# Gated product on groups of 128 tokens behind a top-k attention: x stationary, weights moving 384 columns at a time

## The chip, the core and the metric

The kernel runs on one NeuronCore of a Trainium2 chip. The metric is the device time of one execution in microseconds (us), as a median of several runs. The engines are TensorE (PE; its weight loads are listed as PEld), VectorE (DVE), ScalarE (ACT), GpSimd (POOL) and SyncE (SP, which here only starts DMAs).

## What is computed

```
q, k, v: (4, 8, 576, 64) f32      w_a, w_b: (512, 1536)      w_out: (1536, 512)

scores = q @ k.T / 8                                  # per batch and head, 576 x 576
kth = the 32nd largest score of each row
attn = softmax(scores where scores >= kth, else -1e9)
o = attn @ v                                          # (4, 8, 576, 64)
x = o with heads side by side                         # (2304 tokens, 512)
out = ((x @ w_a) * (x @ w_b)) @ w_out                 # (2304, 512)
```

All matrix products but those with the probabilities use operands split in a high and a low part of type fp32r, and three products (high x high, high x low, low x high) are added in PSUM.

## The kernel before, in words

**Attention.** The work comes in 72 units. A unit is one tile of 128 queries for one pair of heads (`p`, 4 pairs in each of 4 batches), or, for the last 64 queries of a batch, the tail tile of two pairs at once; there are 8 such tail units. `ORDER` gives the order of the tiles in each batch. For each unit, TensorE transposes q (L434), makes the scores in two halves (`qk`, L462), VectorE finds the 32 largest values of each row by four rounds of MAX8 and three of MATCH_REPLACE8 (L887, L904) and writes the mask `keep` (L919). GpSimd adds the mask (L810), ScalarE takes exponentials (L655) and normalises (L670), TensorE transposes the row of both heads in a part of 4 and a part of 5 blocks (`transposes`, L484), multiplies with v (`probs_v`, L501), and subtracts the high part of x to get the low one (L512). Keys of a pair are split and transposed in two parts, `preps` (L420), in the slots that `PREP_SLOT` names.

**Slots.** Each engine runs one loop over slots `s`, in an order of work written out by hand: in slot s, TensorE does `probs_v` of unit s-2, queries of unit s+2, scores of unit s+1, and the transposes of unit s-1, while VectorE searches unit s. The steps of the gated product stand between these.

**The product.** Tokens are taken in 9 groups of G = 256. A group is ready when its 8 units are done, so the product begins in slot `MOE0` = 9. For each of 12 blocks F of 128 hidden columns there are three steps: "a" and "b" (L536: the weight block of 128 x 128 is stationary, x of 256 tokens moves, 4 blocks of the model dimension x 3 = 12 matmuls of 256 columns each) give a and b with the hidden dimension on the partitions; "o" (L551: two halves of the tokens x 3 = 6 matmuls of 512 columns) adds h @ w_out into two PSUM banks. Between them ScalarE copies a and b out of PSUM (L694), GpSimd multiplies (L816), ScalarE rounds to `h_hi` (L699), GpSimd subtracts to `h_lo` (L820). The slots hold 4 and 5 steps by turns (`steps_of`); what is left of the 330 steps after the last slot runs in a loop of its own behind it, and there the engines have nothing else.

```
n = 4 * (s - MOE0) + (s - MOE0) // 2
todo = [[n + part - HALF_SLOT] for part in range(4)] + [[n + 4 - HALF_SLOT] if (s - MOE0) % 2 == 1 else []]
```

**Weights.** There are 36 parts of 128 x 512 (`WCH`): 12 of w_a, 12 of w_b, 12 of w_out. In slots 0 to 9, four per slot, SP loads each to `stage`, ScalarE rounds it to `w_hi` (L604), GpSimd subtracts to the low part (L789). The first 18 low parts stay in SBUF (`w_lo`); the low parts of the last two row blocks of w_b and of all of w_out go to a scratch in memory (`store_low`, L336) and come back for every use: `wb_lo` (128 KB per block F, L351) and `wo_lo` (256 KB per F, L343), in rings of two buffers. The same ring `wo_lo` serves the low parts on their way out.

Of the kernel before, what the change touches and what calls it, by code (L numbers as in the profile page):

```python
# [6 lines left out]
def topk_attention_gated_product(nc, q, k, v, w_parts, xs, out):  # L7
# [3 lines left out]
    P = 128  # L11
# [22 lines left out]
    G = 256  # L34
    GT = G // P
    GROUPS = TOKENS // G
    WC = 512
    WCH = w_parts.shape[0]
    WB0 = KB * DFF // WC
    WO0 = 2 * WB0  # L40

# [4 lines left out]
    RING = 2  # L46
    RING_B = 2
# [6 lines left out]
    ORDER = [[0, 1, 2, 3, 4], [0, 4, 1, 2, 3], [0, 1, 2, 4, 3], [4, 0, 1, 2, 3]]  # L54
# [22 lines left out]
    FIRST, LAST = 0, NU + 2  # L77
    NPREPS = 2 * KB * BATCHES
    PREP_SLOT = [-1] * 4 + [p - 2 for p in range(2, KB) for part in range(2)]
    for b in range(1, BATCHES):  # L80
        late = NU
        slots = []
        for p in range(KB - 1, -1, -1):
            n = b * KB + p - KPAIRS
            free = last_unit(n // KB, n % KB) - 1 if n >= 0 else 0
            for part in range(2):
                at = min(first_unit(b, p) - 2, late - 1)
                if at < free:
                    at = late
                slots.append(at)  # L90
                late = at
        PREP_SLOT += slots[::-1]

# [13 lines left out]
    for b in range(1, BATCHES):  # L107
        for p in range(KB):
            V_AT.setdefault(last_unit(b - 1, p) + 3, []).append((b, p))


    NFS = NF * GROUPS
    STEPS = []
    for F in range(NFS + 2):
        STEPS += [("a", F), ("b", F), ("o", F - 2)]
    MOE0 = PER + 1
    MOE_END = LAST
    PARTS = 5
    HALF_SLOT = 2

    def steps_of(s):

        n = 4 * (s - MOE0) + (s - MOE0) // 2
        todo = [[n + part - HALF_SLOT] for part in range(4)] + [[n + 4 - HALF_SLOT] if (s - MOE0) % 2 == 1 else []]
        return [[m for m in part if m >= 0] for part in todo] if s >= MOE0 else [[]] * PARTS

    SLOT_OF = {n: s for s in range(FIRST, MOE_END) for part in steps_of(s) for n in part}
    N_SLOTTED = len(SLOT_OF)

    def o_step(F):  # L130
        return 3 * (F + 2) + 2


    STAGES = 3
    W_AT = [(0, 1), (0, 3)] + [(s, part) for s in range(1, MOE0 + 1) for part in range(4)]
    W_AT = W_AT[:WCH]
    W_SLOTS = W_AT[-1][0] + 1

    def w_of(s, part):
        return [W_AT.index((s, part))] if (s, part) in W_AT else []  # L140

# [4 lines left out]
    with ExitStack() as ctx:  # L146
# [8 lines left out]
        wo_lo = sb("wo_lo", [P, RING, WC], fp32r)  # L155
        wb_lo = sb("wb_lo", [P, RING_B, KB - LKB, P], fp32r)
        stage = sb("stage", [P, STAGES, WC])
        y = stage
# [18 lines left out]
        ab = sb("ab", [P, 2, 2, G])  # L177
        h_hi = sb("h_hi", [P, 2, G], fp32r)
        h_lo = sb("h_lo", [P, 2, G], fp32r)
# [4 lines left out]
        BY = 4  # L184
        ps_ab = ps[:, 6, :].rearrange("p (w t) -> p w t", w=2)
        ps_x = ps[:, 7, :]
# [6 lines left out]
        def keys_in_psum(n):  # L193
            return [ps_45, ps_67, ps_67, ps_t][n] if n < 4 else ps_t
# [23 lines left out]
        ld_wb = [sem(f"ld_wb{n}") for n in range(RING_B)]  # L218
        ld_wo = [sem(f"ld_wo{n}") for n in range(RING)]
        st_wo = [sem(f"st_wo{n}") for n in range(RING)]  # L220
# [29 lines left out]
        ab_done = sem("ab_done")  # L250
        ab_copied = sem("ab_copied")
        h_ready = sem("h_ready")
        h_hi_ready = sem("h_hi_ready")
        h_lo_ready = sem("h_lo_ready")
# [18 lines left out]
        for g in range(GROUPS):  # L273
            pieces = []
            for t in range(GT):
                tokens = TOKEN_OF[g * G + t * P:g * G + (t + 1) * P]
                at = 0
                while at < P:
                    n = 1
                    while at + n < P and tokens[at + n] == tokens[at] + n:  # L280
                        n += 1
                    pieces.append((t, at, n, tokens[at]))
                    at += n
            PIECES.append(pieces)
# [5 lines left out]
        def _(sp):  # L290
# [37 lines left out]
            def load_w(c):  # L328
                if c < WCH:
                    wait(sp, w_lo_done, c - STAGES + 1)  # L330
                    sp.dma_start(stage[:, c % STAGES, :], w_parts[c]).then_inc(ld_w[c % STAGES], 16)

            def store_low(c):
                n = c - LOW
                sp.wait_ge(w_lo_done, c + 1)
                sp.dma_start(xs[n * P:(n + 1) * P, :], wo_lo[:, n % RING, :].bitcast(fp32)  # L336
                             ).then_inc(st_wo[n % RING], 16)

            def load_wo(F):
                wait(sp, o_done, F - RING + 1)  # L340
                f = F % NF
                row = (WO0 - LOW + f) * P
                sp.dma_start(wo_lo[:, F % RING, :].bitcast(fp32), xs[row:row + P, :]  # L343
                             ).then_inc(ld_wo[F % RING], 16)

            def load_wb(F):
                wait(sp, ab_done, F - RING_B + 1)
                f = F % NF
                at = f % (WC // P) * P
                parts = xs[0:(WO0 - LOW) * P, :].rearrange("(k b p) c -> b p k c", k=KB - LKB, p=P)  # L350
                sp.dma_start(wb_lo[:, F % RING_B, :, :].bitcast(fp32), parts[f // (WC // P), :, :, at:at + P]  # L351
                             ).then_inc(ld_wb[F % RING_B], 16)

            def store_y(g):
                wait(sp, y_ready, GT * (g + 1))
                for t, at, n, row in PIECES[g]:
                    sp.dma_start(out[row:row + n, :], y[at:at + n, t, :]).then_inc(st_y, 16)

            def after_step(n):
                F = n // 3  # L360
                if n % 3 == 1 and F + RING_B < NFS:
                    load_wb(F + RING_B)
                F = n // 3 - 2
                if n % 3 == 2 and F >= 0:
                    if F + RING < NFS:
                        load_wo(F + RING)
                    if F % NF == NF - 1:
                        store_y(F // NF)
# [7 lines left out]
            for c in range(STAGES):  # L376
                load_w(c)
# [3 lines left out]
            for s in range(FIRST, LAST):  # L381
                for b, p in V_AT.get(s, []):
                    load_v(b, p)
                load_q(s + 4)
                mine = preps_at(s)
                for part in range(PARTS):
                    for n in steps_of(s)[part]:
                        after_step(n)
                    if part in (2, 3) and len(mine) > part - 2:
                        load_k(mine[part - 2] + 2)  # L390
                    for c in w_of(s, part):
                        if c >= LOW:
                            store_low(c)
                        load_w(c + STAGES)
                if s == MOE0 - 1:
                    for n in range(RING):
                        sp.wait_ge(st_wo[n], 16 * ((WO0 - LOW) // RING))
                    for F in range(RING_B):
                        load_wb(F)
# [569 lines left out]
```

## Time and profile before

| | us |
|---|---|
| median of 3 runs | 875.44 (873.91 to 876.31) |
| time of the profiled execution | 875.8 |
| its span, first to last instruction | 874.0 |
| TensorE busy | 814.9 (93%) |
| VectorE busy | 780.9 (89%) |
| ScalarE busy | 623.4 (71%) |
| GpSimd busy | 455.5 (52%) |
| mean granted clock of TensorE | 0.969 of full speed |

Busy time of TensorE overstates its load, since matmuls overlap in the pipeline: the distance from one start to the next is what a matmul costs in a row of them. The chain that ended last is followed back from the last instruction to what released each step.

### The profile page before, as it was taken

How to read it: one execution, taken by the hardware profiler on the slowest of the kernel's cores; microseconds unless marked ns; L12 is line 12 of the kernel's file. 1: busy time of each engine (PE TensorE's matmuls, PEld its weight loads, DVE VectorE, ACT ScalarE, POOL GpSimd, SP SyncE). 2: the span in 40 equal slices, each digit the busy share in tenths (PEclk: the TensorE clock that was granted, in tenths of full speed). 3: DMA queues.
4: the chain of work that ended last, by engine and by line, in shares of the span. 5: the costliest groups of instructions: out<-in, count | busy, mean ns of one | idle time of the engine just before them, and what ended most of it. 6: DMA issues, size and time to landing. Idle time of an engine off the chain costs nothing.

```text
span 874.0 us, 19133 instructions
## 1 busy us (share of the span) xinstructions
PE 814.9 (93%) x6576; PEld 734.0 (84%) x6576; DVE 780.9 (89%) x1663; ACT 623.4 (71%) x1416; POOL 455.5 (52%) x504
## 2 busy tenths in 40 slices
PE   6666679999999999999999999999999999999997
PEld 4455568889899998898899999898999998898996
DVE  7899999998999999999999999999999999995000
ACT  5787777777877777778777777787777777775222
POOL 2677754555544455555554455655445445544332
PEclk9966689999999999999999999999999999999999
DMA  4635552222522232224422322233323222311332
GB/s 124 152 110 164 194 164 56 75 75 75 147 80 68 73 97 74 73 80 128 107 77 73 91 68 74 73 106 89 95 74 103 68 68 68 91 55 56 109 91 85
DMA packets 133520, 81.48 MB, mean 93 GB/s; under 512 B 82736, under 2 KB 110384, under 8 KB 133424
## 3 DMA queue, kind: packets, MB, share of 16 engines
q1 hardware_dynamic: 132880, 80.12, 33.0%
q8 instruction: 54, 0.88, 0.4%
q14 instruction: 42, 0.34, 0.1%
q10 hardware_dynamic: 544, 0.13, 0.1%
HBM read 70.78 MB, written 9.44 MB: 92 GB/s over the span
## 4 chain that ended last, share of the span: by engine, by line
DVE 51%; PE 31%; issue 10%; ACT 4%; POOL 2%; DMA 1%; SPq 0%; ACTq 0%
DVE work L904 25%; DVE best L887 20%; PE ps L536 12%; PE ps L551 6%; DVE keep L919 6%; PE ps L462 3%; PE ps L501 3%; PE ps L484 2%; PE ps L420 2%; POOL scores L810 2%; PE ps L434 1%; ACT scores L670 1%; ACT q_t L635 1%; DMA k_rows_b<-in_k 1%; PE ps L442 0%
## 5 line engine op out<-in xcount | busy, mean ns | idle before, releaser
L887 DVE MAX8 best<-work 128x8 f32<-128x576 f32 x432 | 304.7, 747 | 0.0
L536 PE MATMUL ps<-x_hi,w_hi 128*128 128x256 f32 x864 | 251.4, 291 | 0.9 <-ACT x_lo L688 0.9
L810 POOL TENSOR_TENSOR scores<-scores,keep 128x576 f32<-128x576 f32 x144 | 214.7, 1510 | 58.5 <-DVE keep L919 58.5
L536 PE MATMUL ps<-x_lo,w_hi 128*128 128x256 f32 x864 | 243.2, 281 | 0.0
L904 DVE MATCH_REPLACE8 work<-best,work 128x576 f32<-128x576 f32 x288 | 212.8, 743 | 0.0
L536 PE MATMUL ps<-x_hi,w_lo 128*128 128x256 f32 x648 | 182.4, 281 | 0.0
L536 PEld LDWEIGHTS ps<-x_hi,w_hi 128*128 128x128 f32 x864 | 163.0, 189 | 2.2 <-ACT x_lo L688 1.4
L820 POOL TENSOR_TENSOR h_lo<-ab,h_hi 128x256 fp32r<-128x256 f32 x108 | 81.0, 750 | 158.5 <-ACT h_hi L699 158.5
L536 PEld LDWEIGHTS ps<-x_lo,w_hi 128*128 128x128 f32 x864 | 163.2, 189 | 0.5
L655 ACT ACTIVATE scores<-scores,neg_max 128x576 f32<-128x576 f32 x144 | 111.9, 778 | 68.0 <-POOL scores L810 67.2
L462 PE MATMUL ps<-k_t,q_t 128*128 128x288 f32 x632 | 121.2, 320 | 4.9 <-ACT scores L643 4.9
L678 ACT COPY probs_t<-ps 128x512 f32<-128x512 f32 (+1 forms) x144 | 93.4, 649 | 42.2 <-PE ps L484 42.1
L536 PEld LDWEIGHTS ps<-x_hi,w_lo 128*128 128x128 f32 x648 | 122.0, 188 | 0.0
L816 POOL TENSOR_TENSOR ab<-ab 128x256 f32<-128x256 f32 x108 | 80.2, 743 | 75.7 <-ACT ab L694 75.6
L484 PE MATMUL ps<-ident,scores 128*128 128x128 f32 x648 | 100.3, 284 | 20.2 <-ACT probs_t L678 12.8
L670 ACT ACTIVATE scores<-scores,inverse 128x576 f32<-128x576 f32 x144 | 113.5, 788 | 3.1 <-DVE inverse L914 2.1
L694 ACT COPY ab<-ps 128x512 f32<-128x512 f32 x108 | 63.4, 587 | 68.6 <-PE ps L536 67.9
L501 PE MATMUL ps<-probs_t,v_rows 128*64 128x128 f32 (+1 forms) x1600 | 103.7, 282 | 9.1 <-ACT probs_t L678 9.1
L501 PEld LDWEIGHTS ps<-probs_t,v_rows 128*64 128x64 f32 x1600 | 85.8, 145 | 28.1 <-ACT probs_t L678 12.4
L643 ACT COPY scores<-ps 128x576 f32<-128x576 f32 x142 | 92.4, 651 | 18.9 <-PE ps L462 16.6
L904 DVE MATCH_REPLACE8 work<-best,scores 128x576 f32<-128x576 f32 x144 | 105.8, 742 | 0.0
L887 DVE MAX8 best<-scores 128x8 f32<-128x576 f32 x144 | 101.8, 747 | 3.3 <-ACT scores L647 3.3
(56 smaller groups left out, 1294.4 us busy)
## 6 DMA issues: line engine op xcount, KB each, us to landing
wo_lo<-x_scratch SPq DMA_DIRECT2D x108, 256.0 KB, 2.7
wb_lo<-x_scratch SPq DMA_DIRECT2D x108, 128.0 KB, 2.2
stage<-in_w SPq DMA_DIRECT2D x36, 256.0 KB, 3.0
q_rows<-in_q SPq DMA_DIRECT2D x142, 64.0 KB, 2.3
x_scratch<-wo_lo SPq DMA_DIRECT2D x18, 256.0 KB, 2.8
v_rows<-in_v SPq DMA_DIRECT2D x32, 128.0 KB, 2.4
out<-stage SPq DMA_DIRECT2D x15, 256.0 KB, 2.7
k_rows_a<-in_k SPq DMA_DIRECT2D x16, 128.0 KB, 2.3
```

The source lines that it names most:

```text
L462: last = mm(ps_s[:, j, :], weights, k_t[:, (b * KB + p) % KPAIRS, at:at + HALF], start=(i == 0), stop=(i == len(terms) - 1))
L484: last = tr(ps_t[:, at - a:at - a + P], row_of(u)[:, at:at + P], ident[:])
L501: last = mm(ps_x[h * D:(h + 1) * D, i * w:(i + 1) * w], v_rows[:, p, block, h * D:(h + 1) * D], probs_t[:, at:at + w], start=(i == 0 and c ...
L536: last = mm(ps_ab[:, which, :], w, x[:, g % 2, kb, :], start=(kb == 0 and i == 0), stop=(kb == KB - 1 and i == 2))
L643: A.copy(scores[:, u % ROWS, :, half * HALF:(half + 1) * HALF], ps_s[:]).then_inc(s_ready, 1)
L655: A.activation(row, row, ACT.Exp, bias=neg_max[:, u % 2, j:j + 1], scale=SCALE, accum_out=sums[:, u % 2, j:j + 1]).then_inc(e_ready, 1)
L670: A.mul(row, row, inverse[:, u % 2, j:j + 1]).then_inc(p_ready, 1)
L678: A.copy(probs_t[:, a:z], ps_t[:, 0:z - a]).then_inc(pt_ready, 1)
L810: V.tensor_tensor(row, row, keep[:, j, :], ALU.add).then_inc(mask_done, 1)
L820: V.tensor_tensor(h_lo[:, (F - 1) % 2, :], ab[:, (F - 1) % 2, 0, :], h_hi[:, (F - 1) % 2, :], ALU.subtract).then_inc(h_lo_ready, 1)
L887: ins = V.max(best[:, u % 2, j, 8 * r:8 * r + 8], src)
L904: V.match_replace(out=work[:, j, :], in_to_replace=best[:, u % 2, j, 8 * r:8 * r + 8], in_values=src, imm_value=NEG).then_inc(chain, 1)
```

## The change

The product works on 18 groups of 128 tokens. The hidden columns are taken in 4 chunks of HC = 384 per group, 72 chunks in all (`NCH`), and exactly one chunk belongs to a slot, beginning with slot `MOE0` = 5 and ending in slot 78. x (128 tokens) is stationary, 384 columns of the weights move, and so a and b come out with tokens on the partitions. Their product must therefore be turned for the last product: three transposes of 128 x 128 on TensorE (`turn_hidden`), from SBUF to PSUM; ScalarE copies the result twice, once rounded to `h_hi`, once as it is to `h`, and GpSimd subtracts. The output of a chunk (`output`) is 9 matmuls of 512 columns into one PSUM bank, two slots after its columns.

In slot s, with n = s - MOE0, TensorE does the output of chunk n-2 at the head of the slot, half of the a columns of chunk n between the two halves of the scores, the other half after the keys, turns chunk n-1, transposes the first part of the probabilities, does the b columns of chunk n, and transposes the second part. All keys of a slot are transposed together, before the second half of the a columns. GpSimd multiplies chunk n-1 right after the masks, then does up to five weight splits, and the remainder `h_lo` of chunk n-1 last.

`wo_lo` and `wb_lo` become one buffer each, of 768 KB and 384 KB per chunk; low parts on their way to memory have two buffers of their own (`leaving`). `stage` has four buffers in place of three. The weights are split in the order in which chunks need them (`W_ORDER`), five per slot in slots 2 to 4 and four in slots 5 to 8. `ORDER` and `PREP_SLOT` are changed: tail units are units 16 to 19 and 52 to 55 (before: 16, 17, 22, 23, 48, 49, 54, 55), and two slots more than before prepare two key parts each.

```diff
-    G = 256
+    G = P
+    HC = 384
+    HB = HC // P
+    NH = DFF // HC
+    NCH = GROUPS * NH
...
-    RING = 2
-    RING_B = 2
-    ORDER = [[0, 1, 2, 3, 4], [0, 4, 1, 2, 3], [0, 1, 2, 4, 3], [4, 0, 1, 2, 3]]
+    ORDER = [[0, 1, 2, 3, 4], [4, 0, 1, 2, 3], [0, 1, 2, 3, 4], [4, 0, 1, 2, 3]]
...
+        PREP_SLOT += [at + n for n in ((-5, -4, -3, -3, -2, -2, -1, -1) if b % 2 else (-6, -5, -4, -3, -2, -1, 0, 1))]
...
+    MOE_END = MOE0 + NCH + 2
+    for cb in range(NCB):
+        W_BASE.append(len(W_ORDER))
+        W_ORDER += [WB0 + kb * NCB + cb for kb in range(LKB, KB)] + [kb * NCB + cb for kb in range(KB)]
+        W_ORDER += [WB0 + kb * NCB + cb for kb in range(LKB)]
+        last = NF if cb == NCB - 1 else (cb + 1) * HB
+        W_ORDER += [WO0 + f for f in range(cb * HB, last)]
+    STAGES = 4
+    W_AT = [(0, 2), (0, 4)] + [(1, m) for m in (0, 1, 2, 4)] + [(s, m) for s in range(2, 5) for m in range(5)]
+    W_AT += [(s, m) for s in range(5, 9) for m in (0, 1, 2, 4)]
...
+            def load_wo(n):
+                wait(sp, o_done, n)
+                if n < NH:
+                    stored_until(W_ORDER.index(WO0 + f + HB - 1))
...
+            def load_wb(n):
+                wait(sp, ab_done[1], n)
...
+            def columns_of(n, which, blocks):
+                if blocks[0] == 0:
+                    wait(pe, ab_copied[which], n)
+                    if n < NH:
+                        pe.wait_ge(w_lo_done, W_BASE[columns_need(n) - 1] + [KB - LKB + KB, 2 * KB][which])
+                if which == 0:
+                    wait(pe, xlo_done, PER * g + (3 if blocks[0] == 0 else PER))
+                for kb in blocks:
...
+                    for m, (x, w) in enumerate(((x_hi, high), (x_hi, low), (x_lo, high))):
+                        last = mm(ps_ab[which], x[:, g % 2, kb, :], w,
+                                  start=(kb == 0 and m == 0), stop=(kb == KB - 1 and m == 2))
...
+            def turn_hidden(n):
+                pe.wait_ge(h_ready, n + 1)
+                wait(pe, ht_copied, n)
+                for b in range(HB):
+                    last = tr(ps_h[:, b * P:(b + 1) * P], ab[:, 0, b * P:(b + 1) * P], ident[:])
...
+            def output(n):
+                pe.wait_ge(h_lo_ready, n + 1)
+                pe.wait_ge(ld_wo, 16 * (n + 1))
+                for b in range(HB):
+                    for m, (x, w) in enumerate(((h_hi, high), (h_hi, wo_lo[:, b, :]), (h_lo, high))):
+                        last = mm(ps_y, x[:, cols], w, start=(f + b == 0 and m == 0), stop=(f + b == NF - 1 and m == 2))
...
+                output(n - 2)
                 probs_v(s - 2)
                 q_transposes(s + 2)
                 qk(s + 1, 0)
-                steps(todo[1])
+                columns_of(n, 0, (0, 1))
                 x_subtract(s - 2)
                 q_subtract(s + 2)
                 qk(s + 1, 1)
...
+                for m in mine:
+                    k_transposes(m)
+                columns_of(n, 0, (2, 3))
+                turn_hidden(n - 1)
                 transposes(s - 1, 0)
+                columns_of(n, 1, (0, 1, 2, 3))
                 transposes(s - 1, 1)
...
+            def copy_hidden(n):
+                A.copy(h_hi[:], ps_h).then_inc(h_hi_ready, 1)
+                wait(act, h_lo_ready, n)
+                A.copy(h[:], ps_h).then_inc(ht_copied, 1)
...
                 masked(s - 1, 0)
                 masked(s - 1, 1)
                 shifts(s)
+                hidden(n - 1)
+                for m in range(2, 5):
+                    weights(s - 1, m)
+                weights(s, 0)
...
+                weights(s, 1)
+                hidden_lo(n - 1)
```

## Rows read from the trace of the kernel before

**Rows 1.** The page: busy time, bytes moved in 40 slices, the chain.

```profile
PE 814.9 (93%) x6576; PEld 734.0 (84%) x6576; DVE 780.9 (89%) x1663; ACT 623.4 (71%) x1416; POOL 455.5 (52%) x504
...
GB/s 124 152 110 164 194 164 56 75 75 75 147 80 68 73 97 74 73 80 128 107 77 73 91 68 74 73 106 89 95 74 103 68 68 68 91 55 56 109 91 85
...
DVE 51%; PE 31%; issue 10%; ACT 4%; POOL 2%; DMA 1%; SPq 0%; ACTq 0%
```

**Rows 2.** Windows: stretch, its length, busy us per engine (instructions), granted clock, DMA.

```profile
66.00:113.00 47.00, 30.27 (x169) 23.75 (x169) 47.00 (x96) 36.09 (x80) 34.09 (x29) 0.64 0.58 186
...
636.00:798.00 162.00, 160.87 (x1344) 146.38 (x1345) 162.00 (x354) 118.93 (x274) 81.29 (x92) 1.00 0.26 74
798.00:874.00 76.00, 68.20 (x477) 62.28 (x473) 0.27 (x2) 21.44 (x46) 24.74 (x32) 0.98 0.30 87
```

**Rows 3.** Groups of instructions: busy us, mean ns of one, idle before.

```profile
L810 POOL TENSOR_TENSOR scores<-scores,keep 128x576 f32<-128x576 f32 x144 | 214.7, 1510 | 58.5 <-DVE keep L919 58.5
...
L820 POOL TENSOR_TENSOR h_lo<-ab,h_hi 128x256 fp32r<-128x256 f32 x108 | 81.0, 750 | 158.5 <-ACT h_hi L699 158.5
...
L694 ACT COPY ab<-ps 128x512 f32<-128x512 f32 x108 | 63.4, 587 | 68.6 <-PE ps L536 67.9
...
L789 POOL TENSOR_TENSOR wo_lo<-stage,w_hi 128x512 fp32r<-128x512 f32 x18 | 22.8, 1277 | 11.9 <-DMA x_scratch<-wo_lo 8.9 <-ACT w_hi L604 2.9
```

**Rows 4.** Timeline of VectorE, the masks of units 8, 29, 33, 37, 63, 71: start, length.

```profile
111.61 1.94 DVE L919 TENSOR_SCALAR keep<-scores,best 128x576 f32<-128x576 f32 x2
...
342.07 0.93 DVE L919 TENSOR_SCALAR keep<-scores,best 128x576 f32<-128x576 f32 x2
...
385.98 1.76 DVE L919 TENSOR_SCALAR keep<-scores,best 128x576 f32<-128x576 f32 x2
...
430.71 1.08 DVE L919 TENSOR_SCALAR keep<-scores,best 128x576 f32<-128x576 f32 x2
...
712.66 0.94 DVE L919 TENSOR_SCALAR keep<-scores,best 128x576 f32<-128x576 f32 x2
...
797.16 0.95 DVE L919 TENSOR_SCALAR keep<-scores,best 128x576 f32<-128x576 f32 x2
```

**Rows 5.** Timeline of TensorE through two plain units.

```profile
704.69 1.31 PE L501 MATMUL ps<-probs_t,v_rows 128*64 128x128 f32 x20
...
708.13 0.22 PE L512 MATMUL ps<-x_hi,neg_ident 128*128 128x128 f32 x1
...
708.36 0.69 PE L462 MATMUL ps<-k_t,q_t 128*128 128x288 f32 x4
...
710.31 0.60 PE L484 MATMUL ps<-ident,scores 128*128 128x128 f32 x4
710.66 0.36 PE L536 MATMUL ps<-x_hi,w_hi 128*128 128x256 f32 x1
...
717.67 0.28 PE L512 MATMUL ps<-x_hi,neg_ident 128*128 128x128 f32 x1
...
718.43 0.80 PE L462 MATMUL ps<-k_t,q_t 128*128 128x288 f32 x4 [0.15 <-ACT scores L643]
...
725.81 0.33 PE L501 MATMUL ps<-probs_t,v_rows 128*64 128x128 f32 x2
```

**Rows 6.** Timeline of TensorE, key transposes in a slot that prepares keys.

```profile
416.34 0.77 PE L420 MATMUL ps<-ident,k_rows_a 128*128 128x128 f32 x5 [0.51 <-ACT q_t L635]
```

**Rows 7.** Timeline of TensorE in the tail.

```profile
831.04 0.28 PE L536 MATMUL ps<-x_hi,w_hi 128*128 128x256 f32 x1
...
833.91 0.40 PE L551 MATMUL ps<-w_hi,h_hi 128*128 128x512 f32 x1
...
835.31 0.28 PE L536 MATMUL ps<-x_hi,w_hi 128*128 128x256 f32 x1
...
868.11 0.47 PE L551 MATMUL ps<-w_hi,h_hi 128*128 128x512 f32 x1 [1.44 <-DMA wo_lo<-x_scratch]
```

**Rows 8.** DMA issues: transfer, count, size, us to landing.

```profile
wo_lo<-x_scratch SPq DMA_DIRECT2D x108, 256.0 KB, 2.7
```

More of the change, by code:

```diff
@@ L73, in last_unit @@
         return max(u for u in range(NU) if UNITS[u][0] == b and p in UNITS[u][2])
-    FIRST, LAST = 0, NU + 2
+    FIRST = 0
     NPREPS = 2 * KB * BATCHES
-    PREP_SLOT = [-1] * 4 + [p - 2 for p in range(2, KB) for part in range(2)]
+    PREP_SLOT = [-1] * 4 + [0, 0, 1, 1]
     for b in range(1, BATCHES):
[L81 to L92, printed above, removed]
+        at = first_unit(b, 0)
+        PREP_SLOT += [at + n for n in ((-5, -4, -3, -3, -2, -2, -1, -1) if b % 2 else (-6, -5, -4, -3, -2, -1, 0, 1))]
+    for n in range(2 * KB, NPREPS):
+        b, p, before = n // 2 // KB, n // 2 % KB, n // 2 - KPAIRS
+        assert PREP_SLOT[n] <= first_unit(b, p) - 2
+        assert before < 0 or PREP_SLOT[n] >= last_unit(before // KB, before % KB) - 1
     def preps_at(s):
@@ L274, in topk_attention_gated_product @@
             pieces = []
[L275 to L283, printed above, removed]
+            tokens = TOKEN_OF[g * G:(g + 1) * G]
+            at = 0
+            while at < G:
+                n = 1
+                while at + n < G and tokens[at + n] == tokens[at] + n:
+                    n += 1
+                pieces.append((at, n, tokens[at]))
+                at += n
             PIECES.append(pieces)
@@ L339, in load_wo @@
[L339 to L352, printed above, removed]
@@ L354, in store_y, with load_w @@
-            def store_y(g):
[L355 to L368, printed above, removed]
+            def load_w(i):
+                if i < WCH:
+                    wait(sp, w_lo_done, i - STAGES + 1)
+                    sp.dma_start(stage[:, i % STAGES, :], w_parts[W_ORDER[i]]).then_inc(ld_w[i % STAGES], 16)
@@ new lines, in stored_until @@
+            def stored_until(last):
+                for n in range(LOWS):
+                    wait(sp, st_w[n], 16 * sum(LEAVING[m] <= last for m in range(n, len(LEAVING), LOWS)))
+            def load_wo(n):
+                if not 0 <= n < NCH:
+                    return
+                wait(sp, o_done, n)
+                f = n % NH * HB
+                if n < NH:
+                    stored_until(W_ORDER.index(WO0 + f + HB - 1))
+                sp.dma_start(wo_lo[:].bitcast(fp32), xs_o[f * P:(f + HB) * P, :].rearrange("(b p) c -> p b c", p=P)
+                             ).then_inc(ld_wo, 16)
@@ L370, in _, with weights @@
+            def weights(s, m):
+                for i in w_of(s, m):
+                    if W_ORDER[i] >= LOW:
+                        store_low(i)
+                    load_w(i + STAGES)
             load_k(0)
@@ L375, in _ @@
             load_q(2)
-            for c in range(STAGES):
-                load_w(c)
+            load_w(0)
+            load_w(1)
             load_k(4)
@@ L417, in k_transposes @@
                 if n >= 2:
-                    wait(pe, kt_ready, n)
+                    wait(pe, kt_ready, n if to is ps_t else n - 1)
+                if n >= 4 and to is not ps_t:
+                    wait(pe, ab_copied[1], PREP_SLOT[n] - MOE0)
                 for b in range(NB - part):
@@ L755, in _ @@
                 copy_scores(s + 1, 0)
-                between(s, 1)
+                weights(s, 1)
                 normalise(s - 1, 0)
@@ L836, in _ @@
                 split_k(n)
-            for s in range(FIRST, LAST):
+            for s in range(FIRST, MOE_END):
                 masked(s - 1, 0)
```

382 lines of the change are left out of this document (169 added, 213 removed).

## The prediction

> **What bounds the kernel now.** I read the page first, then busy time by stretch, then the timelines of VectorE and TensorE, then the tail. The page [rows 1] shows two engines that are nearly full, TensorE at 93% of the span and VectorE at 89%, and the chain gives 51% of the span to VectorE and 31% to TensorE. So neither is the limit throughout. The windows [rows 2] split the span in three parts with different limits.
>
> The first part ends at about 113 us. From 66 to 113 us TensorE is only 30 of 47 us busy and its granted clock averages 0.64 of full, so between its levels of 1.2 and 2.4 GHz, since there is no product work yet. VectorE is full. GpSimd splits the weights.
>
> The second part ends with the last comparison, `keep` of unit 71, at 797.16 + 0.95 = 798.1 us [rows 4]. From 712.66 to 797.16 eight units take 84.50 us, 10.56 us each, and no gap stands between VectorE's instructions: this is its floor per unit. Over the eight units from 342.07 to 430.71, in which keys are prepared, a unit takes 11.08 us. Over the whole 63 units from 111.61 it is 10.88, some 20 us above the floor, and all of these 20 us lie in the stretches that prepare keys or hold tail units.
>
> Is TensorE far from being the limit in a plain unit? Two units go from 704.69 to 725.81, 21.12 us [rows 5]. Its starts there follow each other without a hole but for one place: from the subtraction of x (L512) to the second half of the scores (L462) it takes 0.76 us from 717.67, and 0.23 from 708.13, where nothing is late, and the scores after it lose another 0.12. That is 0.65 us of waiting for ScalarE. So a plain unit holds (21.12 - 0.65) / 2 = 10.24 us of TensorE work, 0.3 us under VectorE's floor. That small margin is what the change spends.
>
> The third part is the tail: 874.0 - 798.1 = 75.9 us, with VectorE idle and TensorE 68.2 of 76 us busy [rows 2]. The product is late there: 4.5 of its steps fit in a unit from unit slot 9 on, so some 40 of 330 steps are left over after the last slot, nine slots' worth.
>
> **The change part by part.** *The width.* Per slot the product does today 1.5 blocks of 128 hidden columns on 256 tokens: 36 matmuls of 256 columns and 9 of 512. After, it is 24 of 384, the same 9 of 512, and 3 transposes. In the tail, starts go from 831.04 to 833.91 for 24 matmuls of 256, 119.6 ns each, and to 835.31 for six of 512, 233 ns each [rows 7]. A matmul of 384 I put midway, 176.5 ns; in proportion to either neighbour it would be 175 to 179. So 36 x 0.1196 = 4.31 us becomes 24 x 0.1765 = 4.24, within -0.11 and 0. Each matmul has a weight load of its own before (6576 of each [rows 1]), and still has. A transpose of 128 by 128 in fp32 takes 0.35 / 4 = 0.088 us (four from 710.31 to 710.66 [rows 5]), three 0.26. The sum is +0.19 us: 10.43 us per plain unit against VectorE's 10.56. The margin of 0.3 becomes 0.1.
>
> The Trainium skill ("TensorE: Matmul & The Clock Gate", Back-to-back issue gap) gives N/2.4 + 2.5 ns for a warm matmul, 162.5 ns at 384 columns. By it the slot would be 0.3 us lighter than I reckon. At 256 it gives 109 where the tail shows 119.6, so I keep the rows.
>
> *The tail.* A group of 128 tokens is ready after 4 units, so the product starts in slot 5, not 9, and goes one chunk per slot: 72 chunks end their columns in slot 76 and their output in slot 78. From the last `keep` at D: slot 72 waits for masks, exponentials and normalising of unit 71 as now (its transposes start about D+6), and ends about D+9.1; slot 73 has output 2.1, probabilities times v 1.24, columns 4.24, turning 0.26 and about 0.7 of waits and switches, to D+17.7. Slots 74 to 76 hold 4.24 + 2.1 + 0.26 plus 0.4 of waits, 7.0 each, to D+38.8. Then output of chunk 70 (2.1), the load of `wo_lo` for chunk 71, its output (2.1), the copy (0.6) and the store (2.7), with 0.5 of hand-overs. `wo_lo` now has one buffer, and a load brings 768 KB only after the output before it. One of 256 KB lands in 2.7 us [rows 8], and already keeps TensorE waiting 1.44 us at the end [rows 7]; 768 KB lies between that and three times it, 8.1. I take 4.9: the bytes at the page's best slice, 194 GB/s, need 4.0, and something is fixed. That gives D+51, against D+75.9 now: -25 us. With 2.7 us it is -27, with 8.1, four times 3.2 more, -12.
>
> *The start.* All slots from 5 to 8 now carry product work and weight splits together. GpSimd per slot: two masks of 1.51, four splits of about 1.28, and product and remainder of 384 columns, each 1.5 x 0.75 = 1.1 [rows 3], with 0.2 for the shift: 10.5 us, before any wait. Lows that leave for memory go through two buffers, and each must be stored before it is reused. I take 12.1 us per slot in place of some 11.2: +3.6. Slots 2 to 4 hold five splits in place of four, 9.6 us of GpSimd: +1. Chunk 2 needs 28 weight parts at a time when GpSimd is just doing the 28th, and `wo_lo` for chunks 2 and 3 can load only when splits 33 and 36 have been stored, one slot before it is used: +3. Part of chunk 0 runs at the low clock, with 3.6 us of matmuls more to pay twice at worst: +1.5. Sum +9, bounds 0 (all of it under VectorE) and +20.
>
> *The slots with keys or tail units*, about 24 after slot 12. TensorE bounds them, so +0.19 is paid in full. The cover between the two halves of the scores falls from a step of 1.4 us to half a column job of 1.06, and key transposes already waited 0.51 us for ScalarE's copy of q [rows 6]; I add 0.1. 24 x 0.3 = +7, bounds -2 and +12.
>
> *The other 39 slots* fit under VectorE by 0.1 us. I charge 0.1 each for what does not fit, +4, bounds 0 and +16.
>
> *Hidden at nothing:* ScalarE copies 384 columns four times per slot where it copied 1.5 x 512 and 1.5 x 256, about +0.4 us, on an engine 71% busy. If it came on the chain, it would be in the 39 slots' upper bound. DMA traffic for lows doubles (384 to 768 KB of `wo_lo` and 192 to 384 KB of `wb_lo` per slot), at a DMA share of 0.26 [rows 2]. q, k and v queue behind it on SP, and are asked for two slots or more ahead.
>
> Sum: 874.0 - 25 + 9 + 7 + 4 = 869.0 us of span. The profiled execution took 875.8, 1.8 more than its span and 0.4 above the median of the runs; so 870.4, rounded to 870.
>
> **The rivals.** *A. TensorE bounds every slot.* The margin of 0.1 us is smaller than one handover, and outputs now wait within the same slot for turning, two copies and a remainder. If a plain slot costs 0.35 us over my sum, 39 of them cost 14 us: 884. For it: TensorE is 160.9 of 162 us busy from 636 to 798 [rows 2]. Against: the output's chain (copies 0.8, remainder 1.1) has 3 us of other work over it. It decides from 0.2 us per slot on; it is the case on the other side.
>
> *B. GpSimd and VectorE collide.* A pair of `keep` takes 0.93 to 0.95 us alone and 1.76 at 385.98 us [rows 4], in a stretch where GpSimd works at that time. The remainder of a chunk now comes last before the masks, just when VectorE compares. If it lands on `keep` in each plain slot, half of that, 0.4 x 39 = 16 us: 886. Against: the second half of the scores can start 4.8 us after a `keep` ends (718.43 against 712.66 + 0.94); then 0.52, half a column job 1.06 and turning 0.5 bring 6.9, ScalarE is free for the two copies about 7.4 and done at 8.2, the remainder ends at 9.3, and the next `keep` begins at 9.6. So it fits by 0.3 us if TensorE isn't late, and B mostly follows A. The Trainium skill ("SBUF — State Buffer", Who interferes with whom) says that a tensor_scalar in a two-port mode and a GpSimd instruction exclude each other for the whole instruction; the trace agrees with its 1.76, and by that rule one collision could cost up to 1.1 us.
>
> *C. Everything hides.* The start costs 3, the key slots 0, the rest 0: 874.0 - 25 + 3 + 1.4 = 853. For it: VectorE has been full in the first part and GpSimd has gaps there.
>
> *D. The gain and the costs cancel:* a start at +14, or loads of 768 KB near 8 us: 875.
>
> **How the numbers follow.** My forecast (863 to 872.8) 0.42, C and what lies between 0.12, D (872.8 to 878) 0.15, A and B 0.31. A measurement of this kernel tells 0.3%, 2.6 us, from no change. Faster 0.54, the same 0.15, slower 0.31. The range runs from 856, near C, to 887, which takes in A and B.
>
> **What would show it.** Right: the last `keep` 15 to 25 us later than 798 and the span's end about 51 us behind it; matmuls of 384 columns 175 to 179 ns apart; slots 5 to 9 over 12 us; plain slots of 10.6 to 10.7. Wrong: plain slots of 11 us with `keep` pairs of 1.3 us and more (A, B), outputs in the tail waiting over 5 us for `wo_lo`, or `keep` 8 at no more than 115 us (C).

## The result and the profile after

The changed kernel takes 865.22 us (864.08 to 867.99, 4 runs) against 875.38 for the kernel before, a ratio of 0.989 with a 95% interval of 0.9862 to 0.9918. The forecast was 870, faster, with a range of 856 to 887. So the change gains 1.1%, clear of the noise and inside the range. The profiled execution has a span of 862.2 us against 874.0, so 11.8 us less.

The page after: busy time per engine and the chain. They answer to [rows 1].

```profile
PE 814.6 (94%) x5928; PEld 734.1 (85%) x5928; DVE 781.6 (91%) x1663; ACT 660.3 (77%) x1488; POOL 442.9 (51%) x432
...
DVE 51%; PE 25%; issue 11%; DMA 4%; ACT 3%; POOL 3%; SPq 1%; ACTq 0%; POOLq 0%
```

Windows after, to hold against [rows 2]: length, busy us of PE, PEld, DVE, ACT, POOL, granted clock, DMA.

```profile
66.00:111.00 45.00, 38.25 (x269) 34.05 (x270) 43.62 (x93) 38.08 (x88) 36.43 (x33) 0.92 0.69 216
118.00:121.00 3.00, 3.00 (x8) 2.32 (x8) 2.59 (x7) 0.34 (x3) 1.62 (x2) 0.50 0.42 158
650.00:810.00 160.00, 159.63 (x1179) 145.30 (x1178) 159.41 (x345) 126.27 (x286) 79.24 (x77) 1.00 0.43 129
810.00:862.20 52.20, 43.34 (x246) 37.08 (x244) 0.17 (x1) 16.08 (x37) 14.23 (x14) 0.96 0.43 136
```

VectorE's masks after, units 8, 9, 10, 23, 24, 29, 33, 34, 70 and 71: start, length. They answer to [rows 4].

```profile
110.42 1.96 DVE L923 TENSOR_SCALAR keep<-scores,best 128x576 f32<-128x576 f32 x2
123.31 0.94 DVE L923 TENSOR_SCALAR keep<-scores,best 128x576 f32<-128x576 f32 x2
137.84 0.93 DVE L923 TENSOR_SCALAR keep<-scores,best 128x576 f32<-128x576 f32 x2
...
284.80 1.70 DVE L923 TENSOR_SCALAR keep<-scores,best 128x576 f32<-128x576 f32 x2
296.14 1.20 DVE L923 TENSOR_SCALAR keep<-scores,best 128x576 f32<-128x576 f32 x2
...
349.24 0.92 DVE L923 TENSOR_SCALAR keep<-scores,best 128x576 f32<-128x576 f32 x2
...
393.80 1.69 DVE L923 TENSOR_SCALAR keep<-scores,best 128x576 f32<-128x576 f32 x2
405.12 1.69 DVE L923 TENSOR_SCALAR keep<-scores,best 128x576 f32<-128x576 f32 x2
...
797.92 0.93 DVE L923 TENSOR_SCALAR keep<-scores,best 128x576 f32<-128x576 f32 x2
808.48 0.93 DVE L923 TENSOR_SCALAR keep<-scores,best 128x576 f32<-128x576 f32 x2
```

And GpSimd's remainder `h_lo` (L842) beside the masks of units 34 and 70:

```profile
405.42 1.07 POOL L842 TENSOR_TENSOR h_lo<-h,h_hi 128x384 fp32r<-128x384 f32 x1 [4.51 <-ACT h L728]
...
796.58 1.02 POOL L842 TENSOR_TENSOR h_lo<-h,h_hi 128x384 fp32r<-128x384 f32 x1 [4.45 <-ACT h L728]
```

These rows give the sum. The last mask ends at 809.4 us, 11.3 later than before (798.1). Behind it stand 862.2 - 809.4 = 52.8 us, where 75.9 stood: 23.1 less. And 11.3 - 23.1 is the -11.8. Of the 11.3 us, 4.1 are lost by the mask of unit 10 (137.84 against 133.75 before), and 7.2 in all the units after it. Most plain units still take 10.56 us (808.48 - 797.92): VectorE's floor has not moved. There the remainder is done before the masks begin (796.58 + 1.02 against 797.92). A unit in the stretch with keys takes 11.32 (405.12 - 393.80); the remainder runs inside its mask pair, which takes 1.69 us. Some plain units are long too: 11.34 us from unit 23, with a pair of 1.70, to unit 24.

TensorE in a plain slot after: two runs of a columns, the second half of the scores, the turning (L557), transposes, b columns. It answers to [rows 5] and [rows 7].

```profile
729.15 0.34 PE L546 MATMUL ps<-w_hi,x_hi 128*128 128x384 f32 x1
...
730.26 0.33 PE L451 MATMUL ps<-q_t,neg_ident 128*128 128x256 f32 x1
...
730.95 0.34 PE L546 MATMUL ps<-w_hi,x_hi 128*128 128x384 f32 x1
...
732.00 0.49 PE L557 MATMUL ps<-ident,ab 128*128 128x128 f32 x3
732.33 0.60 PE L493 MATMUL ps<-ident,scores 128*128 128x128 f32 x4
732.69 0.42 PE L546 MATMUL ps<-w_hi,x_hi 128*128 128x384 f32 x1
...
740.77 0.33 PE L451 MATMUL ps<-q_t,neg_ident 128*128 128x256 f32 x1
```

Six matmuls of 384 columns start at 730.95 and the next work at 732.00: 175 ns each, near the 176.5 put in the sum. The same instruction comes back 10.51 us later (730.26, 740.77), and no start in between waits. TensorE's work in a plain slot is thus 10.5 us, 0.05 under VectorE's floor, where I had reckoned 10.43.

TensorE's waits for `wo_lo`, in slot 9 and for the last output, and the transfer itself (size, median us to landing; compare [rows 8]).

```profile
114.04 0.74 PE L493 MATMUL ps<-ident,scores 128*128 128x128 f32 x5
117.70 0.66 PE L574 MATMUL ps<-w_hi,h_hi 128*128 128x512 f32 x1 [2.92 <-DMA wo_lo<-x_scratch]
118.16 0.63 PE L574 MATMUL ps<-wo_lo,h_hi 128*128 128x512 f32 x1
118.58 0.63 PE L574 MATMUL ps<-w_hi,h_lo 128*128 128x512 f32 x1
...
855.42 0.76 PE L574 MATMUL ps<-w_hi,h_hi 128*128 128x512 f32 x1 [4.45 <-DMA wo_lo<-x_scratch]
```

```profile
wo_lo<-x_scratch SPq DMA_DIRECT2D x72, 768.0 KB, 4.7
```

The wait of 2.9 us costs twice: after it the matmuls of the output start 0.43 us apart (118.16, 118.58) where they are 0.23 apart at full clock. TensorE was at its lower level, 1.2 GHz, until about 121 us: the granted clock over 118 to 121 us is 0.50, and over 111 to 125 us it averages 0.88.

### The profile page after: what moved, and what is told of

Read it like the earlier page. It is cut to its first block, busy times and chain, and to the rows that moved or that the text cites. A ratio compares the mean times of both kernels' runs of the same rounds, so it can differ in the third digit from the quotient of the medians.

```text
span 862.2 us, 18109 instructions
## 1 busy us (share of the span) xinstructions
PE 814.6 (94%) x5928; PEld 734.1 (85%) x5928; DVE 781.6 (91%) x1663; ACT 660.3 (77%) x1488; POOL 442.9 (51%) x432
## 4 chain that ended last, share of the span: by engine, by line
DVE 51%; PE 25%; issue 11%; DMA 4%; ACT 3%; POOL 3%; SPq 1%; ACTq 0%; POOLq 0%
DVE work L908 25%; DVE best L891 20%; PE ps L546 9%; DVE keep L923 6%; PE ps L574 6%; PE ps L471 3%; PE ps L511 3%; DMA wo_lo<-x_scratch 2%; PE ps L493 2%; POOL scores L828 2%; PE ps L429 2%; POOL leaving L803 1%; PE ps L443 1%; DMA x_scratch<-leaving 1%; PE ps L557 1%
## 5 line engine op out<-in xcount | busy, mean ns | idle before, releaser
L842 POOL TENSOR_TENSOR h_lo<-h,h_hi 128x384 fp32r<-128x384 f32 x72 | 77.5, 1077 | 348.0 <-ACT h L728 348.0
L546 PE MATMUL ps<-w_hi,x_hi 128*128 128x384 f32 x576 | 203.2, 353 | 0.6 <-ACT x_lo L708 0.6
L546 PE MATMUL ps<-w_hi,x_lo 128*128 128x384 f32 x576 | 194.1, 337 | 0.0
L546 PE MATMUL ps<-w_lo,x_hi 128*128 128x384 f32 x432 | 145.7, 337 | 0.0
L471 PE MATMUL ps<-k_t,q_t 128*128 128x288 f32 x632 | 116.7, 311 | 1.2 <-ACT scores L663 1.2
L719 ACT COPY ab<-ps 128x384 f32<-128x384 f32 x144 | 70.7, 491 | 55.9 <-PE ps L546 55.8
L546 PEld LDWEIGHTS ps<-w_hi,x_hi 128*128 128x128 f32 x576 | 108.3, 188 | 2.1 <-ACT x_lo L708 1.2
L546 PEld LDWEIGHTS ps<-w_hi,x_lo 128*128 128x128 f32 x576 | 108.1, 188 | 0.0
L493 PE MATMUL ps<-ident,scores 128*128 128x128 f32 x648 | 96.0, 276 | 12.1 <-ACT probs_t L698 8.1
L574 PE MATMUL ps<-w_hi,h_hi 128*128 128x512 f32 x216 | 92.5, 428 | 10.6 <-DMA wo_lo<-x_scratch 10.5
L471 PEld LDWEIGHTS ps<-k_t,q_t 128*128 128x128 f32 x632 | 92.2, 195 | 3.2 <-ACT scores L663 2.4
```

The lines of the kernel that those rows point to most:

```text
L471: last = mm(ps_s[:, j, :], weights, k_t[:, (b * KB + p) % KPAIRS, at:at + HALF], start=(i == 0), stop=(i == len(terms) - 1))
L493: last = tr(ps_t[:, at - a:at - a + P], row_of(u)[:, at:at + P], ident[:])
L546: last = mm(ps_ab[which], x[:, g % 2, kb, :], w, start=(kb == 0 and m == 0), stop=(kb == KB - 1 and m == 2))
L574: last = mm(ps_y, x[:, cols], w, start=(f + b == 0 and m == 0), stop=(f + b == NF - 1 and m == 2))
```

## The experiments

Each starts from the changed kernel unless said. A diff shows the lines that make the difference; waits, buffer numbers and set-up that follow from them are left out. Times are medians. The kernel before was run again beside each set of kernels, with medians from 873.7 to 875.8 us, and a ratio is taken to the one beside it. To take kernels apart I use the spans of the profiled executions and the end of the last mask, D. Such a comparison has its own noise, of 1 to 2 us and more in the start: kernels that do the same work up to unit 2 have its mask anywhere from 43.0 to 44.5 us.

| kernel | time us | ratio to before (95%) | span | D | behind D |
|---|---|---|---|---|---|
| before | 875.38 | 1 | 874.0 | 798.1 | 75.9 |
| changed | 865.22 | 0.989 (0.9862 to 0.9918) | 862.2 | 809.4 | 52.8 |
| start in slot 9 | 885.5 | 1.013 (1.0113 to 1.0147) | 883.7 | 801.9 | 81.8 |
| start in slot 6 | 867.92 | 0.992 (0.9896 to 0.9945) | 866.4 | 805.6 | 60.8 |
| turned twice | 881.92 | 1.01 (1.0076 to 1.0123) | 880.4 | 825.0 | 55.4 |
| 8 columns of remainder | 859.39 | 0.9842 (0.9811 to 0.9872) | 857.3 | 803.8 | 53.5 |
| turned before keys | 867.48 | 0.9933 (0.9909 to 0.9957) | 865.8 | 812.8 | 53.0 |
| keys later, 8 columns | 870.57 | 0.9958 (0.9934 to 0.9981) | 871.8 | 818.5 | 53.3 |
| before, new order | 879.07 | 1.0045 (1.0026 to 1.0064) | 878.0 | 802.2 | 75.8 |
| `wo_lo` in thirds | 856.5 | 0.979 (0.9763 to 0.9817) | 855.8 | 806.2 | 49.6 |
| thirds, remainder a slot later | 855.39 | 0.9782 (0.9763 to 0.98) | 855.6 | 803.7 | 51.9 |

**The product starts in slot 9.**

```diff
-    MOE0 = PER + 1
+    MOE0 = 9
...
-        leaving = sb("leaving", [P, LOWS, WC], fp32r)
+        leaving = wo_lo
...
-        x_hi = sb("x_hi", [P, 2, KB, G], fp32r)
-        x_lo = sb("x_lo", [P, 2, KB, G], fp32r)
+        x_hi = sb("x_hi", [P, 3, KB, G], fp32r)
+        x_lo = sb("x_lo", [P, 3, KB, G], fp32r)
...
-                    stored_until(W_ORDER.index(WO0 + f + HB - 1))
+                    stored_until(WCH - 1)
```

> The product starts in slot 9 instead of 5, everything else as in the changed kernel. It needs a third buffer for x, and for its room the low parts leave through the buffer of wo_lo. If the gain comes from the earlier start (my forecast), four more slots of about 7 us stand in the tail, 52.8 + 28 = 81 us, while slots 9 and 10 lose the 5 us that they stalled on weights: last mask near 803 to 805, time near 865 + 28 - 5 = 888. Rival: the gain comes from the new form itself (fewer, wider matmuls, regular slots). Then the tail grows but the time stays within 8 us of 865.

Measured: 885.5 us, slower than the kernel before. Behind D stand 81.8 us (81 expected), and D is 7.5 us earlier (5 expected). VectorE's masks of units 7, 8 and 9, in the slots that held product work and weight splits together:

```profile
99.97 0.93 DVE L923 TENSOR_SCALAR keep<-scores,best 128x576 f32<-128x576 f32 x2
110.53 0.93 DVE L923 TENSOR_SCALAR keep<-scores,best 128x576 f32<-128x576 f32 x2
121.09 0.93 DVE L923 TENSOR_SCALAR keep<-scores,best 128x576 f32<-128x576 f32 x2
```

They are 10.56 us apart, where the changed kernel has 11.40 and 12.89 for units 8 and 9. So the early start is the gain: four slots are worth 29 us behind the last mask and cost 7.5 ahead of it. With the start as late as before, the new form of the product with its order of tiles is 9.7 us of span slower than the old one: 3.8 in D, which the order alone accounts for (a run below), and 5.9 behind it. The rival, that the form gains, falls.

**The product starts in slot 6** (`MOE0 = PER + 2`).

> The product starts in slot 6 in place of 5. By the run with slot 9, a slot later costs 7.2 us in the tail, and four of them gave back 7.5 us in the start. If that comes from the weights being late for chunks 2 and 3, one slot more is enough to give most of it, 5 of 7.5: 865.2 + 7.2 - 5 = 867. Rival: it is given back in proportion, 2 us a slot: 870.5.

Measured: 867.92 us. D is 3.8 us earlier, the part behind it 8.0 longer. One slot gives back half of the 7.5 us, between the 5 of my theory and the 2 of the rival. Unit 10 falls from 14.53 to 10.67 us and unit 9 stays at 12.94, so one of the two stalls is gone. The time is not clearly apart from that of the changed kernel (the two intervals overlap), so a start in slot 6 is no gain.

**Each chunk is turned twice.**

```diff
-                for b in range(HB):
+                for b in [b for again in range(2) for b in range(HB)]:
```

> Each chunk's product is turned twice, 6 transposes in place of 3: +0.26 us of TensorE per slot. The trace shows 10.51 us of TensorE work in a plain slot against VectorE's 10.56. If that margin is as thin as it looks, plain slots go from 10.56 to 10.77, some 45 of them, +9 us, and the time is near 874 to 876. Slots with keys stay at 11.33 if the collision of GpSimd and VectorE bounds them. Rival: waits within the slot hide it, as TensorE's busy time is full of overlap: under 3 us, 868 or less.

Measured: 881.92 us, 16.7 more than the changed kernel, and more than I expected. Plain units are 10.84 to 10.87 apart:

```profile
726.21 0.93 DVE L923 TENSOR_SCALAR keep<-scores,best 128x576 f32<-128x576 f32 x2
737.05 0.93 DVE L923 TENSOR_SCALAR keep<-scores,best 128x576 f32<-128x576 f32 x2
```

The margin is as thin as the trace said: nearly all that is added shows. Two things were under-sized. The six transposes take 0.65 us in this kernel's slots, from their start to the next work's, against 0.33 for three: 0.11 us each and not 0.088. And the slots with keys went from 11.33 to 11.58 on average, with mask pairs of 0.93, so here TensorE bounds them.

**The remainder is left out but for 8 columns** (the low part of the hidden values is then missing).

```diff
-                V.tensor_tensor(h_lo[:], h[:], h_hi[:], ALU.subtract)
+                V.tensor_tensor(h_lo[:, 0:8], h[:, 0:8], h_hi[:, 0:8], ALU.subtract)
```

> GpSimd subtracts only 8 of 384 columns of the remainder h_lo; the other columns are zero, so the low part of the hidden values is left out. Theory of the collision: in the slots with keys the remainder (1.08 us) lies under the masks of VectorE, whose pair takes 1.69 instead of 0.92 us, and 10.56 + 0.77 = 11.33 us is just the period seen. Without it these slots are bound by TensorE at about 11.0: 0.35 for some 12 slots plus 0.77 for the four others with long masks (23, 24, 59, 60) and 1 us in the tail, -6 to -8 us. Rival: TensorE bounds the slots with keys and the long masks only fill VectorE's spare time: at most -2 us.

Measured: 859.39 us, -5.8. VectorE's masks in the stretch with keys:

```profile
377.87 0.93 DVE L924 TENSOR_SCALAR keep<-scores,best 128x576 f32<-128x576 f32 x2
389.16 0.93 DVE L924 TENSOR_SCALAR keep<-scores,best 128x576 f32<-128x576 f32 x2
400.36 0.93 DVE L924 TENSOR_SCALAR keep<-scores,best 128x576 f32<-128x576 f32 x2
```

The size came near, the place did not. The masks are short, but the slots are still 11.29 and 11.20 us: VectorE waits there for TensorE's slots of 11.25, and the collision adds 0.08 to each, not 0.35. Even that is not kept: over all units with keys or tails the gain is nothing, since units 16 and 52 now take 12.8 us in place of 11.7 and 11.6. The 5.6 us of D come from elsewhere: 2.9 by unit 12, in the slots with weight splits, where two traces differ by 1 to 2 us anyway; 2.1 at units 23, 24, 59 and 60, whose long masks are gone; and 0.08 in each of the slots right after tail units, 10.59 in place of 10.67. I read those 10.67 us as a loop, from turning over the copies, the remainder, the masks and the exponentials back to TensorE; that they go with the remainder is shown, the loop itself is not.

**Turned before the keys are transposed.**

```diff
                 if mine:
+                    wait(pe, xlo_done, min(s - 1, NU))
+                    turn_hidden(n - 1)
                     wait(pe, qt_ready, min(s + 3, NU))
...
-                wait(pe, xlo_done, min(s - 1, NU))
-                turn_hidden(n - 1)
+                if not mine:
+                    wait(pe, xlo_done, min(s - 1, NU))
+                    turn_hidden(n - 1)
...
+                if mine:
+                    copy_hidden(n - 1)
                 for m in mine:
                     copy_k(m)
...
-                copy_hidden(n - 1)
+                if not mine:
+                    copy_hidden(n - 1)
```

> Only in slots with keys: the product is turned before the key transposes, and ScalarE copies it before the keys. The remainder then comes about 1.1 us earlier and clears the masks. Theory of the collision: masks fall from 1.69 to 0.93 there, the period from 11.33 to 11.0, -4 to -6 us, time near 860. Rival: TensorE bounds these slots at 11.3 anyway, or keys that come later delay the scores: 864 to 867.

Measured: 867.48 us, 2.3 more than the changed kernel, and no gain. The masks of units 33 and 34 stay at 1.68 us and 11.32 apart (394.06, 405.38); the next ones are 11.37, 11.35 and 11.47 apart. Four slots with two key parts take 13.2 us in place of 12.8, and units 16 and 52 take 13.0 in place of 11.7 and 11.6. The first units of the two later stretches do come free: unit 31 takes 10.56 us in place of 11.33, units 50 and 51 10.56 in place of 11.21 and 11.33. But the mask pair of unit 32 is long again, 1.71. It fits TensorE being the bound there: it falls behind VectorE slot by slot, until the remainder meets the masks again. My theory falls with it.

**The keys later, on top of the 8 columns** (low part left out as above).

```diff
+                columns_of(n, 0, (2, 3))
                 if mine:
                     wait(pe, qt_ready, min(s + 3, NU))
                 for m in mine:
                     k_transposes(m)
-                columns_of(n, 0, (2, 3))
...
+                normalise(s - 1, 1)
                 for m in mine:
                     copy_k(m)
-                normalise(s - 1, 1)
```

> As the run with 8 columns of the remainder (the low part of the hidden values is left out), and in slots with keys TensorE does the second half of the a columns ahead of the key transposes, ScalarE the keys after both normalisings. There the slots with keys took 11.20 and 11.29 us with masks of 0.93, so TensorE bounds them, with about 0.2 of waiting for q. Theory: the wait goes, 11.25 falls to 11.05, some 16 slots, -3 us: 856. Rival: the keys are then late for ScalarE and for the first part of the probabilities, which wait in turn: no gain or a loss, 859 to 863.

Measured: 870.57 us, 11.2 more than with 8 columns alone, and units in the stretch with keys 11.54 and 11.76 apart. In the traces D is 14.7 us later: 9.3 in the three stretches with keys or tails, and 5.4 at units 8 to 10, where no keys are prepared. So the price of the edit may be nearer 9 us. TensorE, timeline, one slot of it:

```profile
409.93 0.71 PE L429 MATMUL ps<-ident,k_rows_a 128*128 128x128 f32 x5
410.48 0.49 PE L557 MATMUL ps<-ident,ab 128*128 128x128 f32 x3
411.47 0.63 PE L493 MATMUL ps<-ident,scores 128*128 128x128 f32 x4 [0.50 <-issue]
```

The rival holds, and costs more than it said: the wait of 0.2 us for q is gone, and in its place the transposes of the probabilities start 0.99 us after the turning instead of 0.33. I take the releaser to be ScalarE's copy of the keys, which shares these banks; the trace only says "issue".

**The kernel before with the new order and key slots.**

```diff
-    ORDER = [[0, 1, 2, 3, 4], [0, 4, 1, 2, 3], [0, 1, 2, 4, 3], [4, 0, 1, 2, 3]]
+    ORDER = [[0, 1, 2, 3, 4], [4, 0, 1, 2, 3], [0, 1, 2, 3, 4], [4, 0, 1, 2, 3]]
...
+        PREP_SLOT += [at + n for n in ((-5, -4, -3, -3, -2, -2, -1, -1) if b % 2 else (-6, -5, -4, -3, -2, -1, 0, 1))]
```

> The kernel before with only the new order of tiles (tail units 16 to 19 and 52 to 55) and the new slots for preparing keys. My forecast charged the stretches with keys and tail units 7 us more after the change, all of it to TensorE's heavier slots and shorter cover. If so, the order by itself costs nothing: 873 to 876, and the masks of units 13 to 23 and 49 to 59 take the 11.0 us on average that they take before. Rival: piling two key parts and a tail unit on one slot costs by itself: slots of over 12.4 us four in a row, and +2 to +5 us.

Measured: ratio 1.0045 (1.0026 to 1.0064). The masks of units 17, 18 and 19, after 14.7 us for unit 17 alone:

```profile
213.08 0.94 DVE L909 TENSOR_SCALAR keep<-scores,best 128x576 f32<-128x576 f32 x2
225.24 0.93 DVE L909 TENSOR_SCALAR keep<-scores,best 128x576 f32<-128x576 f32 x2
237.87 1.00 DVE L909 TENSOR_SCALAR keep<-scores,best 128x576 f32<-128x576 f32 x2
```

D is 4.1 us later: some 4.6 us more in the two stretches where two key parts and tail units share slots, less 0.6 ahead of unit 10. The rival holds in its cost, though only units 17 and 19 are over 12.4 us. The order is needed by the change: the tails of two batches, 64 tokens each, must fill one group of 128 together, or a full tile would straddle two groups.

**`wo_lo` in three transfers.** Each third is asked for when its third of the output before is done.

```diff
-                wait(sp, o_done, n)
...
+                for b in range(HB):
+                    wait(sp, o_done, HB * (n - 1) + b + 1)
+                    if n < NH:
+                        stored_until(W_ORDER.index(WO0 + f + b))
+                    sp.dma_start(wo_lo[:, b, :].bitcast(fp32), xs_o[(f + b) * P:(f + b + 1) * P, :]
+                                 ).then_inc(ld_wo[b], 16)
```

> wo_lo comes in three transfers of 256 KB, each asked for as soon as the third of the output before it is done, in place of one of 768 KB. Theory: TensorE's waits for wo_lo (1.6 + 1.1 + 2.9 us in slots 7 to 9, which also set the granted clock down, and 0.5 + 4.3 in the tail) are on the path: slots 9 and 10 fall from 12.9 and 14.5 to about 12, -3 to -4 us, and the tail shortens by 2 to 2.5 us, to 50.5. Time near 859.5. Rival: the start waits for the splits themselves, so that only the tail gains: 863. More transfers on the queue could also delay q: 865 or more.

Measured: 856.5 us, better than expected. The masks of units 8, 9 and 10, and the one wait for `wo_lo` in that slot:

```profile
112.27 1.98 DVE L924 TENSOR_SCALAR keep<-scores,best 128x576 f32<-128x576 f32 x2
123.96 0.93 DVE L924 TENSOR_SCALAR keep<-scores,best 128x576 f32<-128x576 f32 x2
134.62 0.94 DVE L924 TENSOR_SCALAR keep<-scores,best 128x576 f32<-128x576 f32 x2
```

```profile
115.76 0.47 PE L575 MATMUL ps<-w_hi,h_hi 128*128 128x512 f32 x1 [0.46 <-DMA wo_lo<-x_scratch]
```

Units 9 and 10 take 11.69 and 10.66 us in place of 12.89 and 14.53, which is 5.1 less; mask 8 comes 1.9 later in this trace, so D is 3.2 us earlier. The part behind it is 3.2 shorter: the last output now waits 2.29 us for its remainder and not 4.45 for `wo_lo`. The transfer of 768 KB was on the path at both ends, and the rival, that the start waits for the splits themselves, falls.

**The remainder a slot later, on top of the thirds** (the full result).

```diff
-                output(n - 2)
+                output(n - 3)
...
                 hidden(n - 1)
+                hidden_lo(n - 2)
...
-                hidden_lo(n - 1)
```

> On top of the three transfers for wo_lo: the remainder of a chunk moves from GpSimd's end of a slot to the next slot, behind masks, shift and product, where VectorE runs no comparison, and the output follows one slot later (h_hi has two buffers). The full result is computed. Leaving out the remainder gave -5.8 us against the changed kernel: long masks and the 10.67 us loop after tail units were gone. Theory: the same is to be had by moving it, 856.5 - 5 = 851 to 852, with slots 20 to 23 at 10.58, all masks after slot 12 at 0.93 to 0.95 and slots with keys at 11.25; the tail keeps its length, as it only shifts outputs behind columns, +1 at most. Rival: with the product and the remainder right behind the masks, GpSimd splits weights and keys 1.1 us later, the start loses 3 us or more, and nothing is left: 855 to 858.

Measured: 855.39 us, ratio 0.9782 (0.9763 to 0.98), not to be told from the thirds alone (0.9763 to 0.9817). The gain in the middle is there and is spent again at the end. All masks after slot 12 are short, slots with keys take 11.20 and 11.29, and D is 2.5 us earlier. The part behind D is 2.3 us longer: three outputs now follow the last columns in place of two, the second of them waits 1.09 and 0.99 us for `wo_lo`, and the last 1.42 us for its remainder.

## Why the prediction was right

The forecast was a gain in the tail of 25 us less costs of 20, so -5 of span. Measured are -23.1 and +11.3, so -11.8. The way the gain comes about was right, and so nearly was its size; the costs were put too high, which is why 870 came out as 865.2.

**The tail, -25 us.** Right in mechanism and nearly in size: -23.1. The parts listed in the forecast add up to D+51.7 and not D+51, so it should have read -24. The transfer of 768 KB took 4.7 us, where I took 4.9 between bounds of 2.7 and 8.1. The runs with starts in slots 6 and 9 show that it is the start that moves the tail, by 7.2 to 8 us a slot. Not counted was the clock: after its wait of 4.45 us the last output ran in part at the lower level and took 3.6 us instead of 2.1.

**The width.** 175 ns per matmul against 176.5. The neighbours' rows were the better guide than the page's formula ("TensorE: Matmul & The Clock Gate", Back-to-back issue gap, in the Trainium skill), which gives 162.5 for a matmul by itself; the trace, where each matmul has a weight load, does not agree with that number.

**The turning.** Mis-sized: 0.33 us, not 0.26. Four transposes in 0.35 us, as I read them, leave out that the second matmul after them starts 0.08 late. Slot work is 10.51 and not 10.43.

**The start, +9.** Measured +4.1 by unit 10, and made up otherwise than I said. The step that failed is "12.1 us per slot in place of some 11.2" for slots 5 to 8, with its +3.6 and the +1 and +1.5 beside it: those units took 11.25, 11.08, 11.32 and 11.40, and the mask of unit 8 even began 1.2 us earlier than before (110.42 against 111.61), no more than two traces differ by. GpSimd, 36.4 of 45 us busy from 66 to 111 us, did fit its work and its waits for stores into them. The waits for `wo_lo` after late splits, +3, came and were larger: units 9 and 10 took 5.3 us more than before (12.89 + 14.53 against 11.57 + 10.57), and the thirds took nearly all of that away. The trace shows the granted clock at 0.92 from 66 to 111 us, against 0.64 before over the like stretch [rows 2], since product work fills TensorE there; I had put the clock down as a cost only.

**The slots with keys or tail units, +7.** They cost +4.0: after unit 10 they stand 23.1 us over the floor of 10.56 a unit (units 13 to 19, 31 to 38 and 50 to 55), against 19.1 before. I laid it all on heavier slots and shorter cover, but the order by itself costs the kernel before 4.7 us after unit 10. Only in units 31 to 38, which the order leaves nearly as they were, does the form show a price: 1.8 us in 8 units, or 0.23 each, near the 0.3 I had charged. In the two stretches with tail units the changed kernel loses less than the old one with the new order. Why is not shown.

**The other plain slots, +4.** They cost +3.3 us, and not for my reason. The fit of 0.05 us was enough: most take 10.56, and the run with double turning shows how little was left. What they lose is 0.1 us in each slot right after tail units and in slots 11 and 12, and 1.1 us at each of two pairs of units, 24 and 25, 60 and 61, after long masks. Leaving out the remainder brings it down to 0.2 us, so it is the price of the remainder. Against the forecast of -5 of span the start thus gave back 4.9 us, the slots with keys or tails 3.0 and the plain slots 0.7, and the tail took 1.9.

**Rival A** did not happen, but is true one step further: 0.32 us more per slot cost 16.7 us. **Rival B** came in the slots with keys, each mask pair at 1.69 us, and yet cost 0.08 us a slot there, because TensorE was the next bound just under it; its price was 3 us in plain slots, and perhaps as much in the start. That a pair of 0.93 us grows to 1.69 beside a remainder of 1.08 agrees with the rule that the two exclude each other for a whole instruction ("SBUF — State Buffer", Who interferes with whom, in the Trainium skill). **Rival C**, that everything hides, was right for the start up to unit 8, and the sign I had named for it came: mask 8 at 110.42, under 115.

Of my signs for being right, the 51 us behind the last mask (52.8) and the 175 ns came. The last mask is 11.3 us later and not 15 to 25, slots 5 to 8 are not over 12 us, and plain slots are mostly 10.56 and not 10.6 to 10.7. So the direction is earned: the tail was worked out from rows and came out. That the time came within 5 us is in part luck, since of 20 us of costs 8.7 did not come, and the bounds would have allowed more either way.

## What to carry to other kernels

When two engines are both near full and something is left over behind the last unit, starting the late work earlier is worth a whole slot of work for each slot gained (7.2 to 8 us here), even in a form that is slower by itself; ask first what readiness the start waits for (here a group of 256 tokens). Price a transposing or small step by the distance to the second start behind it, since the first one hides part of its cost. A long mask beside another engine's work is a symptom where a third engine sets the pace: take the suspected work away before moving it, and split a transfer that a single buffer puts between two uses.

## What I had not expected of the hardware

A wait of 2.9 us on TensorE, up to 117.70, was followed by about 3 us at the lower level of the granted clock (0.50 from 118 to 121 us), between stretches at full clock (1.00 from 100 to 114 us). Nine matmuls of 512 columns took 3.8 us to the next start (117.70 to 121.50) instead of 2.3 (103.76 to 106.02), so 1.5 us on top of the wait. The same happened after the wait of 4.45 us before the last output. After the wait of 1.05 us before the output at 103.76 the matmuls were 0.23 us apart and the clock stayed at 1.00.
